# A retention and two gated layers on one core: output weights' place, sums' stores, last chunks and the order of the retention's units changed

## The reference

```python
scores = q @ k.T / sqrt(64)
ret = scores * Dmat            # gamma_h ** (i - j) for i >= j, else 0
x = (ret @ v), heads side by side          # 2304 x 512
h = x @ w_in                               # 512 -> 2048
g = h where h >= 1, 0 where h <= -1, else (h + 1)**2 / 4
x = g @ w_out                              # 2048 -> 512
out = ((x @ w_a) * (x @ w_b)) @ w2_out     # 512 -> 1536 -> 512
```

## Time and profile before

| what | us |
|---|---|
| median of 3 runs (lowest 890.07, highest 892.68) | 890.16 |
| the profiled execution's own time | 892.33 |
| its span | 890.5 |
| PE busy | 867.1 (97%) |
| DVE busy | 514.3 (58%) |
| ACT busy | 348.4 (39%) |
| POOL busy | 182.5 (20%) |

### The profile page before, as it was taken

The page is one execution under the profiler, slowest core; times in us unless marked ns, Lnnn a source line. Parts: engine busy times, 40 slices in busy tenths (PEclk is TensorE's granted clock), DMA queues, the critical chain, the costliest instruction groups (busy, mean ns, idle before and its releaser), DMA issues. The chain is left out here.

```text
span 890.5 us, 14103 instructions
## 1 busy us (share of the span) xinstructions
PE 867.1 (97%) x5520; PEld 828.8 (93%) x5520; DVE 514.3 (58%) x873; ACT 348.4 (39%) x650; POOL 182.5 (20%) x198
## 2 busy tenths in 40 slices
PE   7999999989799999999999999999999999999998
PEld 6989999979799999999999899999999999999996
DVE  4776777566534666345776666774434574434343
ACT  1235565445444444453543444342223242223220
POOL 4652123311322323222453333100000000000000
PEclk9999999989899999999999999999999999999999
DMA  9999466953736444653545575465454855454622
GB/s 350 326 362 350 177 223 220 396 222 114 337 100 244 177 170 174 229 184 131 202 157 210 191 281 209 185 231 209 159 213 166 271 179 213 166 213 166 215 69 71
DMA packets 47665, 188.35 MB, mean 212 GB/s; under 512 B 3568, under 2 KB 16368, under 8 KB 38896
## 3 DMA queue, kind: packets, MB, share of 16 engines
q1 hardware_dynamic: 47456, 187.26, 57.3%
q10 hardware_dynamic: 144, 0.20, 0.1%
HBM read 137.63 MB, written 49.81 MB: 210 GB/s over the span
## 5 line engine op out<-in xcount | busy, mean ns | idle before, releaser
L682 PE MATMUL score_b<-xop_hi,wop 128*128 128x384 f32 x416 | 141.0, 339 | 7.6 <-DMA wop<-w_ops 4.8
L686 PE MATMUL score_b<-xop_hi,wop 128*128 128x384 f32 x416 | 139.9, 336 | 0.0
L684 PE MATMUL score_b<-xop_lo,wop 128*128 128x384 f32 x416 | 139.6, 336 | 0.0
L682 PE MATMUL score_a<-xop_hi,wop 128*128 128x384 f32 x312 | 105.5, 338 | 0.0
L684 PE MATMUL score_a<-xop_lo,wop 128*128 128x384 f32 x312 | 104.8, 336 | 0.0
L686 PE MATMUL score_a<-xop_hi,wop 128*128 128x384 f32 x312 | 104.8, 336 | 0.0
L682 PEld LDWEIGHTS score_b<-xop_hi,wop 128*128 128x128 f32 x416 | 78.3, 188 | 12.5 <-DVE a L947 5.1
L684 PEld LDWEIGHTS score_b<-xop_lo,wop 128*128 128x128 f32 x416 | 78.4, 188 | 1.2
L686 PEld LDWEIGHTS score_b<-xop_hi,wop 128*128 128x128 f32 x416 | 78.4, 188 | 0.0
L1191 ACT ACTIVATE p<-score_b 128x384 f32<-128x384 f32 x52 | 25.5, 490 | 100.6 <-PE score_b L686 100.6
L944 DVE SCALAR_TENSOR_TENSOR prod<-prod 128x384 f32<-128x384 f32 x64 | 37.3, 583 | 40.1 <-ACT prod L1175 40.1
(11 more groups left out here) (166 smaller groups left out, 2102.4 us busy)
## 6 DMA issues: line engine op xcount, KB each, us to landing
wop<-w_ops SPq DMA_DIRECT2D x40, 1792.0 KB, 7.4
w_ops<-wop SPq DMA_DIRECT2D x12, 1792.0 KB, 6.5
kq<-k_q SPq DMA_DIRECT2D x16, 576.0 KB, 7.3
wo_raw<-w_out SPq DMA_DIRECT2D x9, 1024.0 KB, 9.4
kvt<-kv_tok SPq DMA_DIRECT2D x16, 512.0 KB, 6.4
w_ops<-s_op SPq DMA_DIRECT2D x8, 1024.0 KB, 5.7
wo_hi<-w_outs SPq DMA_DIRECT2D x8, 1024.0 KB, 7.3
wo_lo<-w_outs SPq DMA_DIRECT2D x8, 1024.0 KB, 9.4
```

Of the source, the lines that this page charges most:

```text
L682: pe.matmul(o, w[:, 0, at], xop_hi[b][:, k, :], start=(start and k == 0), stop=False, skip_group_check=True)
L684: pe.matmul(o, w[:, 0, at], xop_lo[b][:, k, :], start=False, stop=False, skip_group_check=True)
L686: mm = pe.matmul(o, w[:, 1, at], xop_hi[b][:, k, :], start=False, stop=(k == 1), skip_group_check=True)
```

## The change

Six edits:

1. **Memory.** `gh` and `gl` move from before the weights `w1a` to the end of the first part's memory. `w1a` holds 11 columns' weights in place of 12, so the twelfth (f = 11) is loaded with `w1b`, after the last unit. The two buffers of `wo_hi`, `wo_lo` are interleaved, so that the first lies over `xl`, the gate's scratch and the first of `w1a` only. `ab_raw` and `a0` change places.
2. **Waits that follow from it.** `load_out1(0)` waits for `h_ready` 32, `gl_ready` 32 and `y_done` 17, `load_out1(1)` for `y_done` 19, in place of `y_done` 32 for both. `wop`'s first three loads wait for `y_done` 27, 28 and 30 in place of 25, 27 and 29; the first `xop` roundings for 20 to 24 in place of 18 to 23; `gate_high` of the first gated step for `y_done` 31 and 32.
3. **Sums.** SP stores the sums of p ahead of the load and the slabs of p + 2.
4. **The table** `prep_steps` starts three steps earlier.
5. **Last chunks.** Steps 17 to 20 issue one chunk at each of the two places; before, steps 17 and 18 issued two at each and 19 and 20 none.
6. **Units.** The order is pair 0 of batches 0 and 1, pair 1 of them, and so on; then the same for batches 2 and 3. The decays of pairs 1, 2, 3 are loaded after units 1, 3 and 5. ACT's `split_x` waits accordingly.

```diff
-W1A = 12
+X_START = 4 * HALF + 4 * GROUP * DM
+W1A = 11
+def unit(n):
+    n, r = divmod(n, 2 * PAIRS)
+    return r // 2, 2 * n + r % 2
...
-            wo_hi = [sb(f"wo_hi{i}", [P, GROUP, DM], F32R, second) for i in range(2)]
-            with ExitStack() as s:
-                wo_raw = [sb(f"wo_raw{i}", [P, GROUP, DM], F32, s) for i in range(2)]
-            wo_lo = [sb(f"wo_lo{i}", [P, GROUP, DM], F32R, second) for i in range(2)]
+            for i in range(2):
+                wo_hi.append(sb(f"wo_hi{i}", [P, GROUP, DM], F32R, second))
+                with ExitStack() as s:
+                    wo_raw.append(sb(f"wo_raw{i}", [P, GROUP, DM], F32, s))
+                wo_lo.append(sb(f"wo_lo{i}", [P, GROUP, DM], F32R, second))
...
-            if v < 3 or q >= V1 // 2:
+            if v > V1:
+                n = 8 * (V1 // 2 - 1) + 2 * (v - V1 - 1) + place
+                return [n] if n < SHARES1 else []
+            if v < 3:
                 return []
             return [8 * q + 4 * late + 2 * place + i for i in range(2)]
+        def sums_over(end):
+            return NF1 * (NT - 1) + (end - 8 * TC - 4 * TC - 1) // (2 * W1) + 1
...
-        prep_steps = {(0, 9): 0, (0, 12): 1, (1, 1): 2, (1, 2): 3, (1, 4): 4, (1, 5): 5, (1, 7): 6,
+        prep_steps = {(0, 6): 0, (0, 9): 1, (0, 12): 2, (1, 0): 3, (1, 2): 4, (1, 4): 5, (1, 6): 6,
                       (1, 8): 7}
...
-                    end = XBUF * 2 * SUPER + 2 * WOP * (v + 1)
-                    sp.wait_ge(y_done, NF1 * (NT - 1) + (end - 1) // (2 * W1) + 2)
+                    sp.wait_ge(y_done, sums_over(X_START + XBUF * 2 * SUPER + 2 * WOP * (v + 1)))
...
+                if q == 0:
+                    sp.wait_ge(h_ready, NF1 * NT)
+                    sp.wait_ge(gl_ready, NF1 * NT)
                 if q < 2:
-                    sp.wait_ge(h_ready, NF1 * NT)
-                    sp.wait_ge(y_done, NF1 * NT)
+                    sp.wait_ge(y_done, sums_over(4 * HALF + 2 * GROUP * DM * (q + 1)))
...
-                if n < PAIRS - 1:
-                    sp.dma_start(decays[:, n + 1, :], decays_c[:, n + 1, :]).then_inc(decays_loaded[n + 1], 16)
+                p = n // 2 + 1
+                if n % 2 and p < PAIRS:
+                    sp.dma_start(decays[:, p, :], decays_c[:, p, :]).then_inc(decays_loaded[p], 16)
...
             for p in range(NF1 // 2):
+                store_s(p)
                 if p + 2 < NF1 // 2:
                     load_s(p + 2)
                     store_slabs(p + 2)
-                store_s(p)
```

More of the change, by code:

```diff
@@ L107, in build @@
             xl = sb("xl", [P, KT, TC], F32R, first)
-            gh = sb("gh", [P, RING, TC], F32R, first)
-            gl = sb("gl", [P, RING, TC], F32R, first)
             relu_s = sb("relu_s", [P, TC], F32, first)
@@ L131, in build @@
             s_op = blocks("s_op", 2, 4 * AW, first)
+            gh = sb("gh", [P, RING, TC], F32R, first)
+            gl = sb("gl", [P, RING, TC], F32R, first)
         with ExitStack() as second:
@@ L137, in build @@
             b1 = sb("b1", [P, HALF], F32, second)
-            wo_hi = [sb(f"wo_hi{i}", [P, GROUP, DM], F32R, second) for i in range(2)]
-            with ExitStack() as s:
-                wo_raw = [sb(f"wo_raw{i}", [P, GROUP, DM], F32, s) for i in range(2)]
-            wo_lo = [sb(f"wo_lo{i}", [P, GROUP, DM], F32R, second) for i in range(2)]
+            wo_hi, wo_raw, wo_lo = [], [], []
+            for i in range(2):
[3 more added lines that the diff above has]
+                wo_lo.append(sb(f"wo_lo{i}", [P, GROUP, DM], F32R, second))
             xop_hi, xop_lo = [], []
@@ L154, in build @@
             p5 = sb("p5", [P, HALF], F32, second)
+            ab_raw = sb("ab_raw", [P, 4 * AW], F32, second)
             a0 = [sb(f"a0_{i}", [P, HALF], F32, second) for i in range(2)]
-            ab_raw = sb("ab_raw", [P, 4 * AW], F32, second)
         w1_all, w1_raws = w1a + w1b, w1a_raw + w1b_raw
@@ L500, in _ @@
             for n in range(UNITS):
-                s, p, r = n % SLOTS, n % PAIRS, n // SLOTS + 1
-                if n < PAIRS:
+                s, p, r = n % SLOTS, unit(n)[0], n // SLOTS + 1
+                if n < 2 * PAIRS and n % 2 == 0:
                     pool.wait_ge(decays_loaded[p], 16)
@@ L780, in decay_mask @@
             def decay_mask(n):
-                p = n % PAIRS
-                if n < PAIRS:
+                p, _ = unit(n)
+                if n < 2 * PAIRS and n % 2 == 0:
                     dve.wait_ge(decays_loaded[p], 16)
@@ L1024, in copy_ret @@
             def copy_ret(n):
-                p, b = n % PAIRS, n // PAIRS
+                p, b = unit(n)
                 for g in range(2):
@@ L1033, in split_x @@
                 at, wd = STARTS[j % NT], WIDTHS[j % NT]
-                act.wait_ge(ret_copied, 2 * PAIRS * ((at + wd - 1) // SEQ + 1))
+                last = (at + wd - 1) // SEQ
+                act.wait_ge(ret_copied, 2 * (2 * PAIRS * (last // 2 + 1) - 1 + last % 2))
                 for k in tiles:
@@ L1068, in round_op @@
                 if j == 0:
-                    act.wait_ge(y_done, NF1 * (NT - 1) + (2 * SUPER * (i + 1) - 1) // (2 * W1) + 2)
+                    act.wait_ge(y_done, sums_over(X_START + 2 * SUPER * (i + 1)))
                     act.wait_ge(slabs_stored, 64 * (NF1 // 2))
@@ L1179, in gate_high @@
                 g = [a0[p % 2], a1, b1, prod1][i]
+                if p == 0:
+                    act.wait_ge(y_done, NF1 * NT - 1 + row)
                 if p >= 4:
@@ L1280, in by_pair @@
     def by_pair(a):
-        return np.asarray(a).reshape(UNITS, 2, SEQ, HD)
+        heads = np.asarray(a).reshape(BATCH, PAIRS, 2, SEQ, HD)
+        return np.stack([heads[b, p] for p, b in map(unit, range(UNITS))])
     def feature_major(a):
```

## The result

| | before | changed |
|---|---|---|
| median | 890.12 us (889.49 to 892.68) | 876.31 us (876.03 to 877.94) |
| profiled execution | 892.33 us, span 890.5 | 876.33 us, span 874.5 |

The ratio is 0.984, 95% interval 0.982 to 0.987: 13.8 us less, where 14.0 were forecast (876.2). Three of the mechanisms did what was forecast. One did not: putting the stores first had no part in curing the first stall, which went for another reason than the one I gave most of the room to.

What follows compares the result with a forecast made beforehand. PE was taken as the bound, busy 867.1 of 890.5 us, leaving only idle time and slow stretches to win. Terms: 6.7 + 5.6 + 2.8 + 1.1 - 1.8 = 14.4 us, giving 876.2 us, range 871.5 to 883.

Steps and rivals of the forecast that it cites:

- first stall: At 182 us PE waits for `gl` behind late sums, then runs slow; removing it was to gain 6.7 us.
- added sums: One more rounding and split of sums in the direct part's first half was to lose 1.8 us, ends 0 and 4.
- second stall: At 232 us PE waits for `wop`, then runs slow; earlier `wo` loads were to gain 5.6 of 7.4 us.
- steps 17 to 20: Spreading the last chunks over these steps was to fill PE's short waits in steps 19 to 21: 2.8 us gained.
- start: In the retention, decay loads moved from ahead of keys were to end PE's two waits for POOL's keys: 1.1 us gained.
- the loop's time: From rounding sums through store, load and four POOL sums: 12.7 us, fitting in 16.7 us with 4 to spare.
- Rival A: Queue at its limit, sums stay late and the stall at 182 us stands: 882.9 us, chance 0.10.
- wait for DVE's gate: In step 3 PE was to wait some 1.7 us for step 2's gate, too short for the clock to fall.
- `xl` and the copy: Places near 132 and 144 us where added roundings of sums were to delay PE, 1.3 and 0.5 us.
- the clash with POOL: POOL's sums beside DVE were read as a partial slowing, about 1 us a group, not exclusion for whole instructions.
- Rival D: DVE's and ACT's step period is 15.6 us, so PE stalls in four steps of 11.5: 895.4 us, chance 0.03.

Runs made afterwards that it cites:

- e1: Kernel before with only the stores of sums put ahead of loads and slabs and the new sums table: 885.79 us against 890.31.
- e4: Changed kernel with the first two pairs of `wo` loads again waiting for the end of the direct part: 881.47 us.
- e6: Changed kernel with the last eight chunks again in steps 17 and 18, two at a time and twice a step: 879.92 us.
- e5: Changed kernel with units again one batch after the other and decay loads after units 0 to 2: 877.32 us.
- e3: Changed kernel with the old `prep_steps` table, stores of sums kept in front: 881.49 us.
- e10: Changed kernel with one long POOL addition, its result overwritten, ahead of the sums of p = 4 to 7: 878.32 us, one run.
- e8: Changed kernel with `w1` slabs rounded and split in ACT's and DVE's pauses instead of behind the gate, first half of direct part: 873.46 us.
- e12: Kernel before with slab copies of f = 8 to 15 only 64 columns wide instead of 512, output not the reference's: 883.62 us against 889.56.
- e13: Changed kernel with slabs in pauses, step 2's copies behind its last gate, an earlier relu, op 4 and op 5 split later: 875.11 us.

## Why the prediction was right

| term | forecast | measured |
|---|---|---|
| first stall, less the added sums | 6.7 - 1.8 = 4.9 | 4.5 (e1) |
| second stall | 5.6 | 5.2 (e4) |
| steps 17 to 20 | 2.8 | 3.6 (e6) |
| start | 1.1 | 1.0 (e5) |
| sum | 14.4 | 14.3; 13.8 between the medians |

That the forecast of 876.2 lies within 0.1 us of the median is luck in part. Steps 17 to 20 gave 0.8 more than forecast, the other three terms 0.9 less together, and the four terms measured singly make 0.5 more than the medians differ by; the forecast had also been put 0.4 above what the median less 14.4 would give.

**First stall.** The size was right and so was that it would go. The step that failed on the way is the loop's time, "12.7 us", and with it "that store is what edit 3 moves forward". The rounding of p = 5 began at 155.63 and the sums of p = 7 at 168.51, some 3.3 us before their end at 171.8: 16.2 us. Store and load did not take 7.4 us together but some 9 us each from issue to landing (the load was issued at 159.13, behind the store of 157.96), since the queue was full of slab copies. I had that number, 3.4 MB and 371 GB/s make 9.2 us a pair, and treated it as a risk rather than as the bound. Rival A had the mechanism right (the queue is at its limit); it was wrong that the stall follows from it, since the new table gives the last group a place in the queue some 10 us sooner (168.51 against 178.03 in e3 and 178.88 before). It went well by little: ACT took the last sums at 172.68, 0.9 us after POOL had ended them.

**Second stall.** Right step by step: `wo` loads from 202.14, no wait for `wop`, 1.49 us of wait for DVE's gate where 1.7 were forecast, and no fall of the clock after it (the stretch from 230 holds 60 matmuls):

```profile
227.00 0.44 PE L703 MATMUL score_b<-xop_hi,wop 128*128 128x384 f32 x1 [1.49 <-DVE prod L968]
```

**Added sums.** Forecast 1.8 us. Edits 3 and 4 by themselves give 6.7 - 4.5 = 2.2 in e1, and e8 won 2.9 by taking away all of it and what was there before. The place was too narrow: I named `xl` and the copy, 1.3 and 0.5, which the trace has as 0.9 and 0.4 of idle; the steps ahead of them, where `gl` came 0.8 us late in all, I left out, though the chain's 3.8 us a step against PE's 4.2 can take in only 0.4 us of a 1.2 us rounding in each step. How the clash with POOL works was read wrongly, as e10 showed: the four `xl` of 3.04 us were a group of sums in the way of single operations, and where none meets them they take 1.96, so 1.1 us came back there and not 0.8; the two gate operations that meet the new group lose 0.5 and 0.4, near the 1 us forecast. So it had little effect on the sum.

**Steps 17 to 20, start.** Right; the first was undersized by 0.8 us. In before's trace the steps without chunks lack 18 matmuls, 3.0 us, of which I took 2.8; in e6 the same steps lack 21, since PE's waits there for `prod` (L1009) are 0.62 and 0.54 us, where before's timeline prints none for it. e12, which differs from before in the slab copies alone, has them too (0.60 and 0.53 us), so the new memory and the earlier `wo` loads don't make them; what does is not shown. Rival D has nothing for it: PE has no wait in these steps.

## What to carry to other kernels

- If a chain of transfers is late, divide the bytes of one round by the rate that the profile shows in that stretch. If this is about the round's time, no order of the queue helps; fewer bytes or an earlier first round do.
- Two engines that take turns in one chain leave each other pauses. Work that neither waits for belongs into the pauses, not behind the chain (e8: 2.9 us from moving two calls).
- An operand's work moved later is paid at its own product: look up where the product stands before moving it (e13).

## What was not expected of the hardware

- A DVE operation with two SBUF inputs and a POOL operation that reads SBUF took turns by whole instructions: a DVE operation of 0.56 us took 2.13 beside a POOL operation of 1.98 and ended 0.41 after it (e10). The profile shows such waiting as a longer operation, not as idle time, so the mean of several looks like a partial slowing.
- Waits of 1.5 us did not bring PE's clock down (227.00, changed kernel); waits of 3.0 (e13) and 4.7 us (e4) did.
- Some executions are 2 to 3 us longer than others of the same kernel, by PE pauses in the retention that no wait explains ("issue" in the trace). The profiled one of before has such a pause of 0.96 us at 60.11 and begins the direct part at 68.49, that of e13 at 69.11; the twelve others, old and new order alike, at 65.85 to 67.06. Their cause is open. It is most of why the profiled pair differs by 16.0 us and the medians by 13.8.
